# A two-layer mixture of experts on one Trainium2 core: two tiles of the first expert run from fixed rows, ahead of the last routing steps

## The chip, the core and the metric

One core of one Trainium2 chip. The metric is the device time of one execution in microseconds. Each core has TensorE (matrix products and turns, which are products with the identity), VectorE, ScalarE, GpSimd, SyncE and 16 DMA engines, which serve queues: q1 carries what SyncE issues, q10 what ScalarE issues, q0 what GpSimd issues.

## The reference

```
x   = attention(q, k pooled by 8, v pooled by 8)      # 2304 tokens of 512
lg  = x @ w_gate + log1p(exp(x @ w_noise)) * noise    # 8 experts
top = the two largest of each token, weights by softmax
for each expert e and each token that chose it:
    x2[token] += weight * (relu(x[token] @ w1[e]) @ w2[e])       # 512 -> 1024 -> 512
out = sum over 4 experts of p[e] * (relu(x2 @ w1b[e]) @ w2b[e])
```

## The kernel before

The work has three stages on one core, in one program per engine, tied together by semaphores.

**Stage A** goes over 18 tiles of 128 tokens. TensorE computes scores, turns, values and the gate's logits of a tile (`scores`, `e_turn`, `values`, `x_turn_a`, `logits`), VectorE the maxima, the normalisation (`post`) and, for a group of tiles, the choice of two experts (`select`) and the row of each token in its experts' lists (`places`, from the ranks that TensorE adds up in `ranks`). The groups are tiles 0-3, 4-7, 8-11, 12-14, 15-16 and 17 (`GROUPS`). A list of expert e lies in `x_sorted` in DRAM from row e * CAP + 128 on. GpSimd writes each token tile into it twice, by indirect DMAs (`scatter`, L500), one for each choice; tile t waits for `x_ps`, so that the transfers are spread. A ring of 10 tiles holds x (`x_sb`), with one semaphore per slot (`xs_out`).

When the last group is placed, TensorE adds up the counts (L835), and VectorE computes the first row (L1619-1627), the tile table (L1628-1652: which row each tile begins at), the classes and ranks by which 15 of 18 token tiles are sorted by their last expert (`SORTED`; L1655-1683, TensorE L839-841), the codes of the tiles (L1687-1702: expert, buffer, which pieces of weights to split), how many tiles the first block needs (`done_tiles`) and where each token's results lie in `y_sorted` (`y_places`, signal `posy_ok`).

**Stage B** goes over up to 43 row tiles of the lists (`TILES_B`; of these 40 are real with these inputs). Per tile: load 128 rows (ScalarE's queue, L1191 for tile 0, L1183 for others), turn (L859), split x into a high and a low part (ScalarE `x_hi` L1198, VectorE `x_lo` L1588), `up` (24 products in 3 passes, L878), relu (L1207), turn (L887), split h (`h_hi` L1216, `h_lo` L1708), `down` (24 products, L904), copy (L1719), store (L1223). `b_step(u)` on TensorE is: turn h of tile u, turn x of tile u+2, up of tile u+1, down of tile u. The weights come in four raw pieces of 1 MB per expert, through two buffers (`load_raw` on SyncE, L334, waits for `raw_used`), and are split into a high and a low part: for expert 0 ScalarE's `high_first` (L1147) and VectorE's `low_half` (L1581) do it during stage A, at the steps of `HIGH_AT` and `LOW_AT`; for the others GpSimd's `tile_b` (L638 and L641), piece r at the expert's tile r of the one before. GpSimd begins with this when `posy_ok` and all scatters are in, and after tile 0 it writes six token records in sorted order (`sort_records`, L615), after tile 3 nine more. The up of an expert's first tile waits for all four pieces.

In the gap the order of the programs is written out by hand. TensorE: ranks of the last groups, counts, `order_cols` products, `x_turn(0,0)`, `up(0,0)`, wait for the table, `x_turn(0,1)`, `b_step(0,0)`. VectorE: places, select, places, counts, table, `low_half(3, ...)`, `order`, `x_lo(0,0)`, codes, `x_lo(0,1)`, `done_tiles`, `y_places`, `b_step(0,0)`. SyncE: raw pieces 0 and 1, the probabilities, a fill of the lists' fronts from `w1` (L395), pieces 2 and 3, a fill of the tail of `y_sorted` by DRAM-to-DRAM copies (L401, 8 + 7 tiles of 256 KB), pieces of expert 1 and so on.

**Stage D** is the second layer in three blocks of 6 token tiles, with 7 products of halves in place of 8. The first block starts when 34 tiles (`DONE_TILES`) or fewer are stored; at the end each sorted token tile is written by GpSimd's indirect DMA (`store`, L621), the rest by SyncE's plain ones (L439).

```
            x_turn(0, 0)
            up(0, 0)
            pe.wait_ge(tab_ok, 1)
            x_turn(0, 1)
            for u in range(UNROLL_B):
                b_step(0, u)
```

Of the kernel before, what the change touches and what calls it, by code (L numbers as in the profile page):

```python
# [14 lines left out]
P = 128  # L15
# [22 lines left out]
TILES_B = 2 * N // P + EXPERTS - 1  # L38
# [4 lines left out]
SORTED = N // P - 3  # L43
# [39 lines left out]
def build(nc, q, k, v, w_gates, noise, w1, w2, probs, w1b, w2b, out):  # L83
# [5 lines left out]
    with ExitStack() as ctx:  # L89
# [49 lines left out]
        base8 = sb("list_base", [P, EXPERTS], F32, a_sc)  # L139
        noise_sb = sb("noise_sb", [P, NT, EXPERTS], F32, a_sc)  # L140
# [16 lines left out]
        t44 = sb("t44", [1, 18, TILES_B], F32, a_sc)  # L157
        t44i = sb("t44i", [1, 2, TILES_B], I32, a_sc)
        t448 = sb("t448", [1, 2, TILES_B, EXPERTS], F32, a_sc)
        q_sb = sb("qT", [P, 2, HEADS // 2, PAIR], F32, a_sc)  # L160
        kv = sb("kv_half", [P, 5, CHUNKS * POOL * HD // 2], F32, a_sc)
# [6 lines left out]
        nmax = sb("row_max", [P, 2, HEADS], F32, a_sc)  # L168
        ex = sb("exp_scores", [P, 2, HEADS * KEYS], F32, a_sc)
# [4 lines left out]
        aT = sb("x_sbT", [P, KD, P], F32, a_sc)  # L174
        a_sc.close()
# [68 lines left out]
        posy_ok, y_filled = S("y_positions_ready"), S("y_tail_filled")  # L244

# [29 lines left out]
        N_POOL_CONST = 15  # L275
# [44 lines left out]
        def _(sp):  # L320
# [69 lines left out]
            q_load(3)  # L390
            load_raw(0, 0, 0, None)
# [52 lines left out]
        def _(pool):  # L444
# [28 lines left out]
            pool.iota(jrow[:, :], pattern=[[1, TILES_B]], base=0, channel_multiplier=0,  # L473
                      allow_small_or_imprecise_dtypes=True).then_inc(c_pool, 1)
            pool.iota(jnext[:, :], pattern=[[1, TILES_B]], base=1, channel_multiplier=0,
                      allow_small_or_imprecise_dtypes=True).then_inc(c_pool, 1)
            pool.iota(jfirst[:, :], pattern=[[P, TILES_B]], base=0, channel_multiplier=0,
                      allow_small_or_imprecise_dtypes=True).then_inc(c_pool, 1)
            pool.memset(total_b[:, :, :], 0.0).then_inc(c_pool, 1)
            pool.iota(rec[:, :, REC - 1].bitcast(I32), pattern=[[P, NT]], base=0, channel_multiplier=1  # L480
# [12 lines left out]
            def scatter(g):  # L493
                pool.wait_ge(pos_ok, g + 1)
                first, end = GROUPS[g]
# [128 lines left out]
            def tile_b(g, u):  # L624
# [4 lines left out]
                for r in range(4):  # L629
                    with pool.If(code // (32 << r) % 2 > 0):  # L630
                        nslot = pool.snap((e + 1) % 2, min_val=0, max_val=1)
                        if not (isinstance(j, int) and j == 0):
                            pool.wait_ge(y_ps, first)
# [28 lines left out]
            with pool.Fori(1, SURE_GROUPS - 1) as g:  # L662
                for u in range(UNROLL_B):
                    tile_b(g, u)
# [19 lines left out]
            pool.wait_ge(y_ps, pool.value_load(tab2[0:1, 2:3], min_val=EXPERTS - 1, max_val=TILES_B - 1))  # L684
# [60 lines left out]
        def _(pe):  # L745
# [53 lines left out]
            def ranks(g):  # L799
# [3 lines left out]
                if g:  # L803
                    pe.wait_ge(pos_ok, g)
                dst = rank_cols[:, 0:EXPERTS * size]
                pe.matmul(dst, upper[:, :], mask_b[:, first:end, :], start=True, stop=False, skip_group_check=True)
                for j in range(1, size):
# [4 lines left out]
                          start=False, stop=True, skip_group_check=True).then_inc(rank_ps, 1)  # L812

# [15 lines left out]
            for g, (first, end) in enumerate(GROUPS[:-1]):  # L829
                if end + 3 >= NT + 2:  # L830
                    ranks(g)
# [1092 lines left out]
```

## Time and profile before

| | us |
|---|---|
| median of 3 runs | 1411.35 (1409.48 to 1411.98) |
| the profiled execution | 1418.43 |
| its span | 1416.7 |
| TensorE busy | 1348.5 (95%) |
| VectorE busy | 700.4 (49%) |
| GpSimd busy | 693.4 (49%) |
| ScalarE busy | 394.0 (28%) |

The profile follows one execution. The span is from its first to its last instruction; the execution's own time is 1.7 us more, and it lies 7.1 us over the median of the runs. "Granted clock" is TensorE's, as a share of 2.4 GHz: it is 1.0 or 0.5 at a time, and a stretch shows the mean. L is a line of the kernel, `<-` in brackets names who ended an idle time.

### The profile page before, as it was taken

To read this page: it belongs to the slowest core of one execution; us is meant where nothing else is said; L and a number is where in the kernel's file an instruction comes from. 1 tells how busy PE (TensorE), PEld (TensorE's weight loads), DVE (VectorE), ACT (ScalarE), POOL (GpSimd) and SP (SyncE) were. 2 spreads that over 40 slices of the span, in tenths; PEclk is the share of its full clock that TensorE was granted. 3 is DMA by queue.
4 is the path that set the end of the run, shared out by engine and by line. 5 is a ranking of instruction groups with operands and counts; after the bars stand their busy time and mean duration, and the time that the engine had idled before them with its cause. 6 is when DMAs were issued, how large, how long until landed. Compare 5 with 4: busy or idle time off the path is not lost.

```text
span 1416.7 us, 22026 instructions
## 1 busy us (share of the span) xinstructions
PE 1348.5 (95%) x6985; PEld 1186.7 (84%) x6986; DVE 700.4 (49%) x1292; ACT 394.0 (28%) x736; POOL 693.4 (49%) x464
## 2 busy tenths in 40 slices
PE   5992999999999999999999999999999999999997
PEld 4992788888888888878789889899899899989986
DVE  4786422222121222315876685855555655555564
ACT  2561212122212221413343443422222222222210
POOL 1244398274462928397877676442333222233202
PEclk9995999999999999999999999999999999999999
DMA  9948233252333426212323232210011000000002
GB/s 248 282 166 334 75 128 127 84 163 74 131 99 104 134 70 210 84 60 89 99 75 105 90 104 74 82 53 31 30 45 44 30 30 30 30 30 30 14 0 89
DMA packets 63604, 133.71 MB, mean 94 GB/s; under 512 B 5496, under 2 KB 23048, under 8 KB 63448
## 3 DMA queue, kind: packets, MB, share of 16 engines
q1 hardware_dynamic: 43320, 84.69, 18.5%
q0 software_dynamic: 8272, 26.49, 5.8%
q10 hardware_dynamic: 11952, 21.76, 4.7%
q8 instruction: 33, 0.54, 0.2%
q14 instruction: 27, 0.22, 0.1%
HBM read 108.22 MB, written 30.74 MB: 98 GB/s over the span
## 4 chain that ended last, share of the span: by engine, by line
PE 50%; DVE 2%; issue 1%; ACT 0%; DVEq 0%; ACTq 0%
PE banks L1025 26%; PE banks L998 23%; DVE hD L1809 1%; DVE acc L1852 0%; PE banks L984 0%; DVE block_sums L1826 0%; ACT hD L1337 0%; DVE acc L1855 0%; DVE block_sums L1832 0%; DVE x_ops L1805 0%; ACT acc L1227 0%; DVE block_sums L1823 0%; DVE x_sums L1786 0%; ACT unit_w L1359 0%; DVE block_sums L1820 0%
## 5 line engine op out<-in xcount | busy, mean ns | idle before, releaser
L1025 PE MATMUL banks<-unit_w,hD 128*128 128x512 f32 x1728 | 404.7, 391 | 3.2 <-DVE acc L1852 2.5
L1025 PEld LDWEIGHTS banks<-unit_w,hD 128*128 128x128 f32 x1728 | 322.2, 188 | 73.0 <-DVE acc L1852 7.1
L998 PE MATMUL banks<-x_ops,unit_w_hi 128*128 128x384 f32 x1344 | 342.3, 335 | 5.9 <-issue 2.6
L998 PEld LDWEIGHTS banks<-x_ops,unit_w_hi 128*128 128x128 f32 x1344 | 243.3, 188 | 11.5 <-issue 5.4
L1852 DVE SCALAR_TENSOR_TENSOR acc<-banks,sorted_record,acc 128x512 f32<-128x512 f32 x270 | 200.5, 748 | 104.4 <-PE banks L1025 101.5
L878 PE MATMUL banks<-expert_w,xT 128*128 (+1 forms) x960 | 230.7, 396 | 1.5 <-DVE xT L1588 1.5
L533 POOL TENSOR_TENSOR unit_w_lo<-raw_weights,unit_w_hi 128x512 fp32r<-128x512 f32 (+1 forms) x60 | 63.1, 1072 | 339.4 <-ACT unit_w_hi L1353 339.3
L904 PE MATMUL banks<-expert_w,hT 128*128 (+1 forms) x960 | 226.3, 392 | 2.7 <-issue 2.7
L998 PE MATMUL banks<-x_ops,unit_w_lo 128*128 128x384 f32 x672 | 225.1, 335 | 0.0
L904 PEld LDWEIGHTS banks<-expert_w,hT 128*128 128x128 f32 x960 | 181.2, 189 | 40.6 <-issue 3.0
L878 PEld LDWEIGHTS banks<-expert_w,xT 128*128 128x128 f32 x960 | 178.4, 189 | 38.5 <-issue 2.2
L1719 DVE COPY y_rows<-banks 128x512 f32<-128x512 f32 x40 | 27.7, 692 | 331.9 <-PE banks L904 331.9
L638 POOL TENSOR_TENSOR expert_w<-raw_weights,zeros 128x2048 f32 x28 | 100.8, 3600 | 168.6 <-PE banks L904 135.8
L641 POOL TENSOR_TENSOR expert_w<-raw_weights,expert_w 128x2048 f32 x28 | 128.8, 4602 | 5.2 <-POOL expert_w L638 5.2
L998 PEld LDWEIGHTS banks<-x_ops,unit_w_lo 128*128 128x128 f32 x672 | 126.1, 188 | 0.0
L1809 DVE SCALAR_TENSOR_TENSOR hD<-block_sums,hD 128x384 fp32r<-128x384 f32 x144 | 95.6, 692 | 28.6 <-ACT hD L1337 28.5
L1216 ACT CAST hT<-banks 128x512 fp32r<-128x512 f32 x80 | 43.0, 590 | 189.5 <-PE banks L887 189.5
L1207 ACT ACTIVATE h_rows<-banks 128x512 f32<-128x512 f32 x80 | 43.5, 595 | 180.4 <-PE banks L878 162.3
L537 POOL TENSOR_TENSOR unit_w<-raw_weights,unit_w 128x1024 fp32r<-128x1024 f32 x31 | 75.7, 2442 | 27.6 <-ACT unit_w L1359 27.6
L1335 ACT COPY block_sums<-banks 128x384 f32<-128x384 f32 x48 | 23.0, 480 | 205.1 <-PE banks L998 200.0
L1708 DVE TENSOR_TENSOR hT<-banks,hT 128x512 fp32r<-128x512 f32 x80 | 51.5, 686 | 49.1 <-ACT hT L1216 47.7
L533 POOL TENSOR_TENSOR unit_w_lo<-weight_sums,unit_w_hi 128x1024 fp32r<-128x1024 f32 x30 | 73.9, 2464 | 0.0
(232 smaller groups left out, 1278.0 us busy)
## 6 DMA issues: line engine op xcount, KB each, us to landing
raw_weights<-in_w SPq DMA_DIRECT2D x32, 1024.0 KB
raw_weights<-in_w1b SPq DMA_DIRECT2D x32, 512.0 KB
raw_weights<-in_w2b SPq DMA_DIRECT2D x32, 512.0 KB, 3.3
x_rows<-x_sorted ACTq DMA_DIRECT2D x43, 256.0 KB, 2.7
y_sorted<-y_rows ACTq DMA_DIRECT2D x40, 256.0 KB
qT<-in_q SPq DMA_DIRECT2D x3, 1152.0 KB, 23.0
kv_half<-in_k SPq DMA_DIRECT2D x5, 576.0 KB, 12.7
kv_half<-in_v SPq DMA_DIRECT2D x5, 576.0 KB, 12.3
```

Source lines behind the costliest of these rows:

```text
L533: ins = pool.tensor_tensor(lo, src, hi.bitcast(F32), ALU.subtract)
L537: pool.tensor_tensor(w2o[par][:, 1, :], raw[:, par, 1024:2048], w2o[par][:, 0, :].bitcast(F32), ALU.subtract).then_inc(w2_ok, 1)
L638: pool.tensor_tensor(hi, src, zeros[:, 0:1].to_broadcast([P, 2048]), ALU.add).then_inc(split_no, 1)
L641: pool.tensor_tensor(lo, src, hi.bitcast(F32), ALU.subtract).then_inc(raw_used[r % 2], 1)
L878: mm = pe.matmul(bank[n][:, :], xT[:, u % 2, st, c, :], wall[:, bass.ds(slot, 1), 0, mv, FF * c + 512 * n:FF * c + 512 * n + 512], start=( ...
L904: mm = pe.matmul(bank[5 + u % 2][:, :], hT[:, u % 2, st, c, :], wall[:, bass.ds(slot, 1), 1, mv, D * c:D * c + D], start=(t == 0), stop=(t ...
L998: mm = pe.matmul(dst[:, 0:HALF], (w1h, w1l)[st][par][:, b, c, :], x2o[blk][:, a, mv, c, :], start=(first and t == 0), stop=(t == 5), skip_ ...
L1025: mm = pe.matmul(bank[5 + t % 3][:, :], hD[:, buf, st, c, P * t:P * t + P], w2o[par][:, mv, D * c:D * c + D], start=(n == 0), stop=(n == 3 ...
L1207: r = act.activation(h_sb[:, 512 * n:512 * n + 512], bank[n][:, :], ACT.Relu)
L1708: d = dve.tensor_tensor(hT[:, u % 2, 1, 4 * n:4 * n + 4, :], bank[2 + n][:, :].rearrange("p (c r) -> p c r", c=4), hT[:, u % 2, 0, 4 * n:4 ...
L1809: dve.scalar_tensor_tensor(out=hD[:, buf, 1, m, at:at + HALF], in0=src, scalar=0.0, in1=hD[:, buf, 0, m, at:at + HALF].bitcast(F32), op0=A ...
L1852: dve.scalar_tensor_tensor(out=to, in0=bank[5 + t % 3][:, :], scalar=p, in1=to, op0=ALU.mult, op1=ALU.add).then_inc(acc_ok, 1)
```

## The change

Two tiles of expert 0 are taken from the front of its list at fixed rows (128 to 383) and computed with expert 0's weights while the last token tiles are still being routed; the tile table counts from the third tile on. The token tiles 0 to 11 (the first three groups) give these rows. If they have fewer than 256 tokens for expert 0, the rest of the 256 rows stays what a fill wrote (`early_filled`), and later tokens are placed behind (`late_base`, `early_count`). The loads of the two tiles are on SyncE's queue, behind the waits for the scatters of tiles 0 to 11 and ahead of expert 1's raw pieces. There are 45 row tiles in place of 43, 17 sorted token tiles in place of 15. `h_lo`, `y_copy`, `x_lo` of the early tiles stand among VectorE's table operations. Some buffers change places in memory.

```diff
+EARLY = 2
+EARLY_GROUPS = 3
-TILES_B = 2 * N // P + EXPERTS - 1
+TILES_B = 2 * N // P + EXPERTS - 1 + EARLY
-SORTED = N // P - 3
+SORTED = N // P - 1
-        HIGH_AT = {11: 0, 14: 1, 17: 2, 19: 3}
+        HIGH_AT = {11: 0, 14: 1, 17: 2}
 (SyncE)
             q_load(3)
+            sp.dma_start(x_sorted[P:P + EARLY_ROWS, :]..., w1[1]...[0:EARLY_ROWS, :]).then_inc(early_filled, 16)
             load_raw(0, 0, 0, None)
...
             load_raw(3, 0, 3, 1)
-            for i, (first, end) in enumerate(((DONE_TILES - 6, DONE_TILES + 2), (DONE_TILES + 2, TILES_B))):
+            for i, (first, end) in enumerate(((DONE_TILES - 6, DONE_TILES + 2), (DONE_TILES + 2, TILES_B - 1), (TILES_B - 1, TILES_B))):
                 sp.dma_start(y_sorted[first * P:end * P, :], w1[i]...).then_inc(y_filled, 16)
+            sp.wait_ge(sc_ps, NT)
+            for i in range(XS):
+                sp.wait_ge(xs_out[i], 32 * len(range(i, EARLY_TOKENS, XS)))
+            for j in range(EARLY):
+                sp.dma_start(xg[:, j, :], x_sorted[P + P * j:2 * P + P * j, :]).then_inc(xg_in[j], 16)
             with sp.Fori(1, EXPERTS) as e:
 (GpSimd)
                 pool.wait_ge(pos_ok, g + 1)
+                if g == 0:
+                    pool.wait_ge(early_filled, 16)
...
-            tile_b(0, 0)
-            pool.wait_ge(order_ok, 1)
-            pool.wait_ge(wts_ok, len(GROUPS))
-            pool.wait_ge(p_ok, 2)
-            sort_records(0, 6)
-            for u in range(1, UNROLL_B):
+            for u in range(EARLY, UNROLL_B):
                 tile_b(0, u)
-            sort_records(6, SORTED)
+            for g, (first, end) in enumerate(((0, 6), (6, 12), (12, SORTED))):
+                for u in range(UNROLL_B):
+                    tile_b(g + 1, u)
+                if g == 0:
+                    pool.wait_ge(order_ok, 1)
+                    pool.wait_ge(wts_ok, len(GROUPS))
+                    pool.wait_ge(p_ok, 2)
+                sort_records(first, end)
 (TensorE)
+                if s == EARLY_TOKENS + 4:
+                    early_count()
             x_turn(0, 0)
+            for g, (first, end) in enumerate(GROUPS[:-1]):
+                if end + 3 >= NT + 2:
+                    ranks(g)
             up(0, 0)
+            ranks(len(GROUPS) - 1)
+            x_turn(0, 1)
+            h_turn(0, 0)
+            count()
+            up(0, 1)
+            order()
+            down(0, 0)
+            h_turn(0, 1)
+            down(0, 1)
+            x_turn(0, EARLY)
             pe.wait_ge(tab_ok, 1)
-            x_turn(0, 1)
-            for u in range(UNROLL_B):
+            codes[EARLY] = load_code(pe, EARLY)
+            up(0, EARLY)
+            x_turn(0, EARLY + 1)
+            for u in range(EARLY, UNROLL_B):
                 b_step(0, u)
 (ScalarE)
             x_hi(0, 0)
+            high_first(3)
+            for g, (first, end) in enumerate(GROUPS):
+                if end + 3 >= NT + 2:
+                    second_exp(g)
+            relu(0, 0)
+            x_hi(0, 1)
+            h_hi(0, 0)
+            relu(0, 1)
+            h_hi(0, 1)
...
+            act.dma_start(xg[:, EARLY, :], x_sorted[bass.ds(row, P), :]).then_inc(xg_in[EARLY], 16)
             act.wait_ge(rows_ok, 1)
-            x_load(0, 1)
-            relu(0, 0)
-            x_load(0, 2)
-            x_hi(0, 1)
-            x_load(0, 3)
-            for u in range(UNROLL_B):
-                b_step(0, u, start=True)
+            x_load(0, EARLY + 1)
+            y_store(0, 0)
+            for u in range(EARLY):
+                x_load(1, u)
+            x_hi(0, EARLY)
+            x_hi(0, EARLY + 1)
+            relu(0, EARLY)
+            for u in range(EARLY, UNROLL_B):
+                b_step(0, u)
 (VectorE)
+            def late_base():
+                dve.wait_ge(early_ps, 1)
+                then(dve.tensor_tensor(bump8[:, 0, :], early8[:, :], count_cols, ALU.subtract))
+                then(dve.tensor_scalar(bump8[:, 0, :], bump8[:, 0, :], 0.0, None, ALU.max))
+                dve.tensor_tensor(base_late[:, :], base8[:, :], bump8[:, 0, :], ALU.add)
...
+                dve.sem_inc(early_ok, 1)
...
+                if s == EARLY_TOKENS + 5:
+                    late_base()
...
             for g in late:
                 places(g)
+            x_lo(0, 0)
             select(len(GROUPS) - 1)
+            low_half(3, 0)
             places(len(GROUPS) - 1)
+            x_lo(0, 1)
...
             dve.tensor_copy(first_row[:, :], front[0:1, 0:1]).then_inc(first_ok, 1)
+            low_half(3, 1)
+            h_lo(0, 0)
...
-            for half in range(2):
-                low_half(3, half)
...
             dve.tensor_copy(order_i[:, :], order_f).then_inc(order_ok, 1)
-            x_lo(0, 0)
+            h_lo(0, 1)
+            y_copy(0, 0)
...
-            x_lo(0, 1)
             done_tiles()
             y_places()
-            b_step(0, 0)
+            y_copy(0, 1)
+            x_lo(0, EARLY)
+            x_lo(0, EARLY + 1)
+            b_step(0, EARLY)
```

## Rows read from the trace of the kernel before

**Rows 1.** Busy time by stretch; columns PE, PEld, DVE, ACT, POOL, clock, DMA share, GB/s.
```profile
113.00:141.00 28.00, 3.63 (x30) 3.20 (x30) 17.75 (x73) 2.67 (x7) 11.90 (x12) 0.50 0.90 341
...
117.85:157.10 39.25, 13.90 (x71) 11.00 (x72) 21.29 (x95) 4.09 (x8) 8.09 (x9) 0.63 0.57 210
```

**Rows 2.** Timeline of TensorE; start, length, engine, line, count, idle before.
```profile
141.32 1.11 PE L859 MATMUL banks<-ident,x_rows 128*128 128x128 f32 x4 [10.14 <-DMA x_rows<-x_sorted]
...
155.18 5.74 PE L878 MATMUL banks<-expert_w,xT 128*128 x24
...
160.76 5.61 PE L904 MATMUL banks<-expert_w,hT 128*128 128x512 f32 x24
...
204.16 2.09 PE L878 MATMUL banks<-expert_w,xT 128*128 x8
```

**Rows 3.** Timeline of GpSimd, from the scatters to the fourth weight piece.
```profile
111.85 0.97 POOL L500 DMA_INDIRECT x_sorted<-x_sb,pos_int  x1 [0.30 <-issue]
...
127.40 0.97 POOL L500 DMA_INDIRECT x_sorted<-x_sb,pos_int  x1 [0.30 <-issue]
...
158.54 3.60 POOL L638 TENSOR_TENSOR expert_w<-raw_weights,zeros 128x2048 f32 x1 [30.17 <-issue]
...
194.15 3.60 POOL L638 TENSOR_TENSOR expert_w<-raw_weights,zeros 128x2048 f32 x1
197.94 4.61 POOL L641 TENSOR_TENSOR expert_w<-raw_weights,expert_w 128x2048 f32 x1 [0.19 <-POOL expert_w L638]
```

**Rows 4.** Timeline of VectorE: last selection, a low part of h, a copy.
```profile
117.89 0.18 DVE L1500 TENSOR_TENSOR noisy_logits<-noisy_logits,noise_sb 128x8 f32<-128x8 f32 x1
...
157.01 1.28 DVE L1708 TENSOR_TENSOR hT<-banks,hT 128x512 fp32r<-128x512 f32 x2
...
166.40 0.69 DVE L1719 COPY y_rows<-banks 128x512 f32<-128x512 f32 x1 [7.52 <-PE banks L904]
```

**Rows 5.** Waits of VectorE from 117.8 to 157.2; total, times, longest.
```profile
DVE xT L1588 <- ACT xT L1198: 10.7, 2, 5.8
DVE total_b L1519 <- DVE group_total L1516: 1.2, 1, 1.2
DVE cnt L1635 <- DVE cnt L1633: 1.0, 1, 1.0
```

**Rows 6.** Groups by line, 141 to 151.2 us: busy, mean ns, idle before.
```profile
L878 PE MATMUL banks<-expert_w,xT 128*128 128x512 f32 x24 | 7.3, 470 | 1.5 <-DVE xT L1588 1.5
```

**Rows 7.** Timeline of the DMA issues: y fill on SyncE, tile 0 on ScalarE.
```profile
106.25 1.73 SPq L401 DMA_DIRECT2D y_sorted<-in_w  x2
...
136.49 0.40 ACTq L1191 DMA_DIRECT2D x_rows<-x_sorted  x1
```

**Rows 8.** DMA queues, 100 to 106 us; packets, MB, share of 16 engines.
```profile
q0 software_dynamic: 240, 0.79, 34.5%
```

**Rows 9.** DMA queues, 110 to 122 us.
```profile
q1 hardware_dynamic: 263, 4.27, 94.7%
q0 software_dynamic: 121, 0.43, 9.3%
...
x_sorted<-x_sb,pos_int POOLq DMA_INDIRECT x9
```

**Rows 10.** DMA queues, 122 to 127 us, and time to landing.
```profile
q1 hardware_dynamic: 264, 1.00, 48.6%
q0 software_dynamic: 276, 0.91, 45.3%
...
x_sorted<-x_sb,pos_int POOLq DMA_INDIRECT x4, 9.0
```

**Rows 11.** Busy time by stretch around an early wait of TensorE, columns as in rows 1.
```profile
32.00:34.00 2.00, 0.49 (x4) 0.49 (x5) 0.10 (x1) 0.00 (x0) 0.00 (x0) 1.00 0.98 220
34.00:36.00 2.00, 2.00 (x13) 1.76 (x12) 1.23 (x2) 0.00 (x0) 0.00 (x0) 0.66 1.05 232
```

**Rows 12.** Timeline of the last stores.
```profile
1408.20 2.45 SPq L439 DMA_DIRECT2D out<-acc  x3
```

More of the change, by code:

```diff
@@ L631, in tile_b @@
                         nslot = pool.snap((e + 1) % 2, min_val=0, max_val=1)
-                        if not (isinstance(j, int) and j == 0):
-                            pool.wait_ge(y_ps, first)
+                        pool.wait_ge(y_ps, first)
                         src = raw[:, r % 2, :]
@@ L661, in _ @@
                            records[2 * BLOCK:SORTED * P, :].rearrange("(p t) r -> p (t r)", p=P)).then_inc(recs_in, 16)
-            with pool.Fori(1, SURE_GROUPS - 1) as g:
+            with pool.Fori(4, SURE_GROUPS - 1) as g:
                 for u in range(UNROLL_B):
@@ L812, in ranks, with early_count, count, order @@
                           start=False, stop=True, skip_group_check=True).then_inc(rank_ps, 1)
+            def early_count():
+                pe.wait_ge(tot_ok, EARLY_GROUPS)
+                pe.wait_ge(pos_ok, EARLY_GROUPS)
+                pe.matmul(count_cols, ones_b[:, :], total_b[:, EARLY_GROUPS % 2, :],
+                          start=True, stop=True).then_inc(early_ps, 1)
+            def count():
+                pe.wait_ge(tot_ok, len(GROUPS))
+                pe.wait_ge(pos_ok, len(GROUPS))
+                pe.matmul(count_cols, ones_b[:, :], total_b[:, len(GROUPS) % 2, :],
+                          start=True, stop=True).then_inc(cnt_ps, 1)
+            def order():
+                pe.wait_ge(class_ok, 1)
+                pe.matmul(order_cols, upper[:, :], class_b[:, :, :], start=True, stop=False, skip_group_check=True)
+                for j in range(1, SORTED + 1):
+                    mm = pe.matmul(order_cols[:, EXPERTS * j:], ones_b[:, :], class_b[:, 0:SORTED + 1 - j, :],
+                                   start=False, stop=j == SORTED, skip_group_check=True)
+                mm.then_inc(order_ps, 1)
             scores(0)
@@ L1169, in _ @@
                     high_first(HIGH_AT[s])
-            for g, (first, end) in enumerate(GROUPS[:-1]):
-                if end + 3 >= NT + 2:
-                    second_exp(g)
             softplus(len(GROUPS) - 1)
-            second_exp(len(GROUPS) - 1)
             codes = {}
@@ L1232, in first_copy, with b_step @@
                 act.copy(acc[1][:, n, :], first_bank(n)[:, :]).then_inc(x2T_ok, 1)
-            def b_step(g, u, start=False, rows=((), (), ())):
+            def b_step(g, u, rows=((), (), ())):
                 j = UNROLL_B * g + u
@@ L1239, in b_step @@
                 h_hi(g, u)
-                if not (start and u == 0):
-                    y_store(g if u else g - 1, (u - 1) % 4)
+                y_store(g if u else g - 1, (u - 1) % 4)
                 x_hi(g + (u + 2) // 4, (u + 2) % 4)
@@ L1589, in x_lo, with h_lo, y_copy @@
                                   xT[:, u % 2, 0, :, :].bitcast(F32), ALU.subtract).then_inc(bxT_lo, 1)
+            def h_lo(g, u):
+                j = UNROLL_B * g + u
+                dve.wait_ge(hT_hi, j + 1)
+                for n in range(2):
+                    d = dve.tensor_tensor(hT[:, u % 2, 1, 4 * n:4 * n + 4, :],
+                                          bank[2 + n][:, :].rearrange("p (c r) -> p c r", c=4),
+                                          hT[:, u % 2, 0, 4 * n:4 * n + 4, :].bitcast(F32), ALU.subtract)
+                d.then_inc(hT_lo, 1)
+            def y_copy(g, u):
+                j = UNROLL_B * g + u
+                dve.wait_ge(y_ps, j + 1)
+                if not (isinstance(g, int) and g == 0 and u < 2):
+                    dve.wait_ge(y_out[u % 2], 16 * (2 * g + u // 2))
+                dve.tensor_copy(y_sb[:, u % 2, :], bank[5 + u % 2][:, :]).then_inc(y_ok, 1)
             kv_pool(0, 0)
@@ L1696, in _ @@
             then(dve.tensor_copy(t44[:, 8, :], t44i[:, 1, :]))
+            then(dve.scalar_tensor_tensor(out=t44[:, 1, :], in0=behind[:, :, 0], scalar=float(EARLY), in1=t44[:, 1, :],
+                                          op0=ALU.mult, op1=ALU.add))
             then(dve.tensor_scalar(t44[:, 1, :], t44[:, 1, :], 1.0, None, ALU.max))
@@ L1757, in _ @@
             domain_weights()
-            for u in range(1, UNROLL_B):
+            for u in range(EARLY + 1, UNROLL_B):
                 b_step(0, u)
```

116 lines of the change are left out of this document (59 added, 57 removed).

## The prediction

> **What bounds the kernel now.** I read the windows of the start first: from 113 to 141 us TensorE works 3.63 us of 28 at a granted clock of 0.50, and from 141.3 on it multiplies with few breaks [rows 1, 2]. Whatever the change gives it must take from this gap, because the first expert network, once under way, runs at TensorE's pace: from the up of tile 1 (155.18, 5.74 us) to that of tile 5 (204.16) are four tiles, so 12.24 us each, of which up and down take 11.35 and turns the rest; two tiles are worth 24.5 us [rows 2]. Tile 5 is the first of expert 1; by its up both kernels have done the same products, and from there on they do the same, so **the start of up(5) is the mark by which I measure the change**.
>
> Three chains meet in the gap. VectorE goes from the last group's selection (117.89) to the y positions (done at 157.1) [rows 1, 4], but waited 10.7 us of these 39.2 for x, which TensorE turns and ScalarE casts [rows 5]. GpSimd issues scatters until 128.4, then waits for the y positions, and its four pieces of expert 1's weights begin at 158.54 and end at 202.55, 1.6 us before the mark [rows 3]. The queues are the third: the tile load is issued only at 136.49 though the last scatter was issued at 127.40, and TensorE can turn it at 141.3 [rows 2, 3, 7]. The DMA views say why. Up to 106 the scatter queue q0 had moved three scatters (0.79 MB of 0.26 each). The y fill is issued at 106.25; from 110 to 122 q1 moves 4.27 MB and q0 0.43 MB, though GpSimd had issued nine scatters in it; only from 122 on do they share (1.00 and 0.91 MB in 5 us) [rows 7 to 10]. Eight scatters, tiles 0 to 11's last, are 2.10 MB from 100 us on, and q0 reaches 0.79 + 0.43 + 0.91 = 2.13 MB at 127. So **tile 11's scatter, issued at 111.85, has landed only at about 127**.
>
> **The change, part by part.** The first two tiles are taken off the gap's end and put ahead of `ranks(4)` on TensorE, but they need rows that scatters of tiles 0 to 11 wrote.
>
> *When the early rows land (X).* SyncE waits for these scatters behind the y fill. The fill grows from 15 to 17 tiles, 3.75 to 4.25 MB; at q1's 4.27 MB in 12 us that is 1.4 us more, so it ends near 123.4. Against that, the raw load that shared with q0 from 122 is now issued behind the early loads. Alone, q0 gets about both shares, 1.91 MB in 5 us, so its missing 0.83 MB take 2.2 us: 125.6. From the queue's state to a load's issue and from there to TensorE's turn I take before's steps, about 1.0 and 4.8 us (136.49 to 141.32) [rows 2, 7]: X = 131.4, say **131**. Bounds: below, 112.8 + 4 + 2.8 = 119 or so if nothing starved; above, 134 if the three scatters of tile 12 on, already queued, take their full turn ahead.
>
> *From X to the y positions.* Relative to X: turn at half clock 1.1, `ranks(4)` and `places(4)` 1.4, and x's low half, so up(0,0) starts at 3.4 and takes before's 7.3 us for its 24 products, the first 3 us of them at the low clock [rows 6]: 10.7. `ranks(5)` stands behind it, so VectorE, which has finished the last selection and a weight half at 6.2, waits 4.9 us for it; `places(5)` and x's low half of tile 1 end at 13.1 and the counts come in. The steps that follow are small operations of 0.2 to 0.5 us, taken from before's timeline between the ends that the rows give, one by one, without its stalls. The first row 1.5, a weight half 1.2, h's low half of tile 0 1.3 [rows 4], the table's first part and the classes 4.1: 21.2. Meanwhile up(0,1) ended at 18.9 and TensorE stood for `order()`, which waits for the classes. `order()` 1.3 and down(0,0) 5.6 [rows 2] bring it to 28.3, turn and casts to 30.5. VectorE has the order at 26.4 and waits 4.1 us there for h of tile 1: its low half ends at 31.8, the copy of y (0.7) at 32.5 [rows 4], the tile table (4.4) at 37.0, done tiles and y places (1.6 + 2.0 and 0.7 for the added operations) at **X + 41.3**. The check from the other side: 39.2 - 10.7 us of waits = 28.5; VectorE's waits on itself while GpSimd issued scatters (1.2 and 1.0 are the longest [rows 5]) go, since its scatters lie elsewhere now, giving 26.3; added are two h halves 2.6, a copy 0.7, the small operations 1.1 and the two new waits 4.9 + 4.1: 39.7 from X + 2.5 on, 42.2, within 1 us of the other.
>
> *To the mark.* GpSimd starts 1.45 us after the positions (157.1 to 158.54) and splits four pieces at 8.37 us (194.15 to 202.55 holds one) without the six record scatters that lay between before: X + 41.3 + 1.45 + 33.5 = X + 76.3. TensorE's own way: up(0,2) waits for x's low half, which stands behind the y places and a copy in VectorE's order: X + 42.8, 5.74, the turn of x for tile 3, its cast, relu 2.3, then h's turn at 51.0, and from there two tiles and the turns, 25.7: X + 76.7. The two limits are level, so nothing is had by shortening one. The mark is at 131 + 76.7 = **207.7**, before 204.16: +3.5.
>
> *The clock.* TensorE now waits three times (2.3 us ahead of `order()`, 2.5 ahead of down(0,1), 4.6 ahead of up(0,2)). In the trace two microseconds with 0.49 busy (32 to 34) were followed by a granted clock of 0.66 [rows 11], while between the ups of tiles 0 and 1, which lie 4 us apart, nothing fell. Up(0,0) shows what low time costs: 7.3 us in place of 5.74 [rows 2, 6]. So 1.6 us a fall; I take one, +1.6. Bounds 0 and 4.8. [...]
>
> *The end.* 17 sorted tiles make tiles 3 and 4 of the last block go out by GpSimd's indirect store (about 1 us of issue, slower to land) in place of SyncE's plain ones, from 1408.20 on [rows 12]; the last tile stays plain. Bounds 0 and 1.5, I take 0.6. Two more empty tail steps on each engine, two more record scatters and `order()` products: the first 0.4 (0 to 1), the others lie under tiles with slack. The record scatters move between tiles 7 and 8, 11 and 12, 15 and 16; six are 7.6 us, four pieces 33.5, and five tiles last 61.2, so they fit. `late_base` (six operations, 1.2 us) comes before the last tile's x, and is hidden since X is later than all it delays. The early fill (0.5 MB at about 47 us) pushes weight loads that are needed at 80; free. Real tiles: 40 before; the inputs route 417 rows to expert 0 in its first 12 token tiles, over 256, so 40 again.
>
> Sum: +3.5 + 1.6 + 0.6 + 0.4 = **+6.1 us** on the profiled execution's 1418.4; on the median of the runs, 1411.35 (7 below it), that gives **1417.4**. This kernel's measurement can tell some 0.2%, 2.8 us, from no change.
>
> **The rivals.** (A) *The fill starves nobody when it counts, faster.* The place is SyncE's wait for tiles 0 to 11. The early rows then land at about 119, the chain of 76.7 ends at 195.7, and with a fall and the end the result is 8.5 less and 2.6 more, 5.9 less than 1411.35: 1405.5. The turning point is X = 125 (131 less 6.1). For it: q0 did move 0.43 MB during the fill and the three scatters before the fill were through by 106 [rows 8]. Against: every byte count above. The Trainium skill (DMA: Bandwidth & Descriptors, Anatomy of one DMA) gives a GpSimd-issued transfer 2.0 us and its bytes over 436 GB/s, an estimate of 2.6 us for 256 KB; with it the early rows would be in at 118 and the result near 1404. The trace's own landings of 9.0 us speak against it here [rows 10]. Chance 0.17.
> (B) *The chain is 4 to 5 us shorter than I add up, no change.* VectorE's waits on itself all go, no clock falls, X = 129: 1411 to 1414. Chance 0.20.
> (C) *More falls and a later X, slower still.* X at 134 puts the mark 6.5 later, three falls cost 4.8 and the end 1: 12.3 more than 1411.35, so 1423.7. Chance 0.15.
> (D) *The early tiles are padding or cost an extra tile*: expert 0 short of 256 rows, +12.2 us. Excluded by the 417 but for 0.01.
>
> **How the numbers follow.** The forecast as summed, 1414.2 to 1421, gets 0.47. Slower by over 0.2% is the forecast with (C) and (D), 0.63; same 0.20; faster 0.17. The range must take in part of (A) and most of (C): 1405 to 1423. The likeliest case's own range is 1414 to 1421.
>
> **What would show it.** The early x loads issued by SyncE at 125 to 128 and landing near 131, q0 nearly still until 123; y positions at 170 to 174; the first split piece right behind, four in a row; TensorE with 24 + 24 + 24 + 24 products between 134 and 169 and three waits; the mark near 208 to 210. The forecast is wrong if the first x turn comes before 125, or if up(5) does not stand at GpSimd's fourth piece or within 2 us of it.

## The result and the profile after

The changed kernel takes **1435.15 us** (median of 4 runs, 1430.53 to 1437.79) beside 1411.06 for the kernel before on the same chip: it is slower by 24.1 us. The ratio of the fast runs is 1.0151 (95% interval 1.0126 to 1.0176); the quotient of these two medians is 1.0171. The forecast was 1417.4: the sign came out, the size did not, and the time lies outside the range. The profile is of the fastest of the four runs (1430.53).

The page of the kernel after (its span, the busy tenths of TensorE in 40 slices, its clock):

```profile
span 1428.6 us, 22041 instructions
PE 1352.0 (95%) x6988; PEld 1188.3 (83%) x6989; DVE 711.2 (50%) x1302; ACT 393.6 (28%) x736; POOL 696.8 (49%) x470
...
PE   6995789999999999998999999999999999999997
```

In the stretch of [rows 1], busy time and clock are now these (columns as there):

```profile
113.00:141.00 28.00, 15.55 (x65) 12.44 (x66) 9.31 (x36) 5.22 (x9) 6.10 (x7) 0.67 0.55 213
```

TensorE works 15.55 of the 28 us in place of 3.63. Part of this is chance, since stage A ended some 7 us later in the first trace of before: in the repeated profiles below, the same stretch holds 13.47 in place of 6.10. The gap was filled as intended, and the time still went up. The timeline of TensorE tells where it went:

```profile
123.03 1.11 PE L897 MATMUL banks<-ident,x_rows 128*128 128x128 f32 x4 [14.93 <-DMA x_rows<-x_sorted]
...
125.80 8.39 PE L920 MATMUL banks<-expert_w,xT 128*128 128x512 f32 x24 [1.60 <-DVE xT L1675]
...
153.62 5.70 PE L948 MATMUL banks<-expert_w,hT 128*128 128x512 f32 x24 [2.58 <-DVE hT L1682]
...
164.23 8.00 PE L920 MATMUL banks<-expert_w,xT 128*128 x24 [4.47 <-DVE xT L1675]
...
200.19 7.16 PE L948 MATMUL banks<-expert_w,hT 128*128 x24 [6.48 <-issue]
207.19 1.04 PE L929 MATMUL banks<-ident,h_rows 128*128 128x128 f32 x8
208.42 5.74 PE L920 MATMUL banks<-expert_w,xT 128*128 x24
...
642.52 7.36 PE L948 MATMUL banks<-expert_w,hT 128*128 x24 [2.74 <-issue]
653.00 0.41 PE L1058 MATMUL banks<-x_ops,unit_w_hi 128*128 128x384 f32 x1 [3.12 <-issue]
654.52 0.48 PE L1058 MATMUL banks<-x_ops,unit_w_hi 128*128 128x384 f32 x1 [1.11 <-issue]
```

Three things answer to [rows 2]. The first x turn (X) is at 123.03. Up(5), the mark, is at 208.42, 85.4 us behind X and 4.3 us later than in the first trace of before. And stage D (L1058) does not start at the last down's end but 3.1 us behind it, with a second wait at once. The waits of 2.58 and 4.47 us and the two slow ups are near the forecast (2.5 and 4.6, and one fall of the clock); the 6.48 us ahead of down(3) are not.

The timeline of VectorE beside that wait, and then that of GpSimd:

```profile
186.97 0.69 DVE L1693 COPY y_rows<-banks 128x512 f32<-128x512 f32 x1 [8.51 <-PE banks L948]
187.57 1.80 DVE L1618 TENSOR_SCALAR top_sum<-top_diff_exp 128x2 f32<-128x2 f32 x1
189.40 0.17 DVE L1619 RECIPROCAL token_record<-top_sum 128x2 f32<-128x2 f32 x1
189.60 3.32 DVE L1620 TENSOR_TENSOR token_record<-top_diff_exp,token_record 128x2 f32<-128x2 f32 x1
...
193.22 4.39 DVE L1620 TENSOR_TENSOR token_record<-top_diff_exp,token_record 128x1 f32<-128x1 f32 x1
...
198.71 1.28 DVE L1682 TENSOR_TENSOR hT<-banks,hT 128x512 fp32r<-128x512 f32 x2
```

```profile
184.75 4.59 POOL L667 TENSOR_TENSOR expert_w<-raw_weights,expert_w 128x2048 f32 x1 [0.19 <-POOL expert_w L664]
189.30 3.60 POOL L664 TENSOR_TENSOR expert_w<-raw_weights,zeros 128x2048 f32 x1
193.09 4.50 POOL L667 TENSOR_TENSOR expert_w<-raw_weights,expert_w 128x2048 f32 x1 [0.19 <-POOL expert_w L664]
```

Three operations on one or two numbers per partition take 1.80, 3.32 and 4.39 us, and end at 189.37, 192.92 and 197.61, within 0.03 us of the ends of GpSimd's three splits (189.34, 192.90, 197.59). The low half of h, queued behind them, starts at 198.71, and down(3) needs it.

SyncE's issues in the gap (fill, then the early rows), and at the end the last accumulation and the last store:

```profile
98.19 2.76 SPq L418 DMA_DIRECT2D y_sorted<-in_w  x3
118.61 1.15 SPq L425 DMA_DIRECT2D x_rows<-x_sorted  x2
...
1418.49 0.75 DVE L1950 SCALAR_TENSOR_TENSOR acc<-banks,sorted_record,acc 128x512 f32<-128x512 f32 x1 [0.61 <-PE banks L1085]
1419.27 0.37 SPq L462 DMA_DIRECT2D out<-acc  x1
```

From the last accumulation's end (1419.24) to the span's end are 9.4 us; before it was 6.4.

### The profile page after: what moved, and what is told of

The parts are those of the page before. It is cut to its first block, busy times and chain, and to the rows that moved or that the text cites. A ratio compares the mean times of both kernels' runs of the same rounds, so it can differ in the third digit from the quotient of the medians.

```text
span 1428.6 us, 22041 instructions
## 1 busy us (share of the span) xinstructions
PE 1352.0 (95%) x6988; PEld 1188.3 (83%) x6989; DVE 711.2 (50%) x1302; ACT 393.6 (28%) x736; POOL 696.8 (49%) x470
## 4 chain that ended last, share of the span: by engine, by line
PE 50%; DVE 2%; issue 1%; ACT 0%; POOLq 0%; POOL 0%; DVEq 0%
PE banks L1085 26%; PE banks L1058 24%; DVE hD L1907 1%; DVE acc L1950 0%; PE banks L1044 0%; DVE block_sums L1924 0%; DVE acc L1953 0%; DVE block_sums L1930 0%; DVE x_ops L1903 0%; ACT acc L1275 0%; POOLq L95 0%; DVE x_sums L1884 0%; ACT hD L1402 0%; DVE x_sums L1886 0%; ACT hD L1406 0%
## 5 line engine op out<-in xcount | busy, mean ns | idle before, releaser
L1058 PE MATMUL banks<-x_ops,unit_w_hi 128*128 128x384 f32 x1344 | 343.5, 336 | 9.9 <-issue 6.8
L1058 PEld LDWEIGHTS banks<-x_ops,unit_w_hi 128*128 128x128 f32 x1344 | 244.1, 188 | 14.3 <-issue 9.0
L920 PE MATMUL banks<-expert_w,xT 128*128 (+1 forms) x960 | 234.4, 401 | 6.3 <-DVE xT L1675 6.3
L948 PE MATMUL banks<-expert_w,hT 128*128 (+1 forms) x960 | 228.2, 394 | 11.8 <-issue 9.2
L1058 PE MATMUL banks<-x_ops,unit_w_lo 128*128 128x384 f32 x672 | 225.8, 336 | 0.0
L1058 PEld LDWEIGHTS banks<-x_ops,unit_w_lo 128*128 128x128 f32 x672 | 126.5, 188 | 1.3 <-issue 1.3
```

The lines of the kernel that those rows point to most:

```text
L920: mm = pe.matmul(bank[n][:, :], xT[:, u % 2, st, c, :], wall[:, bass.ds(slot, 1), 0, mv, FF * c + 512 * n:FF * c + 512 * n + 512], start=( ...
L948: mm = pe.matmul(bank[5 + u % 2][:, :], hT[:, u % 2, st, c, :], wall[:, bass.ds(slot, 1), 1, mv, D * c:D * c + D], start=(t == 0), stop=(t ...
L1058: mm = pe.matmul(dst[:, 0:HALF], (w1h, w1l)[st][par][:, b, c, :], x2o[blk][:, a, mv, c, :], start=(first and t == 0), stop=(t == 5), skip_ ...
```

## The experiments

Times are medians; the kernel before had 1411.6, 1412.8 and 1412.1 us in the three sets of runs (e1 to e4; e5, e7, e8, e10; e11 to e14). "From X to the mark", "last down to last accumulation" and "end" are read from each run's timeline as above.

### The two kernels again

No edit. The kernel before, profiled once more:

> The kernel before, profiled a second time, to see how far its first profiled execution (1418.43 us against a median of 1411.4) speaks for it. Theory A (the first profile had a stage A that was some 7 us too long by chance: last logits at 115.06 against 108.13 in the profile of the changed kernel, whose stage A is the same up to there): the last logits now end near 108, the product of tile 5 that was at 204.16 starts near 197, and the time is near 1411. Theory B (the change itself shortens stage A by some 7 us, through the moved fill or the moved scatters): the last logits end near 115 and the product of tile 5 starts near 204 again.

```profile
134.68 1.11 PE L859 MATMUL banks<-ident,x_rows 128*128 128x128 f32 x4 [15.43 <-DMA x_rows<-x_sorted]
...
199.94 5.73 PE L878 MATMUL banks<-expert_w,xT 128*128 x24
...
633.73 7.35 PE L904 MATMUL banks<-expert_w,hT 128*128 x24 [2.74 <-issue]
640.92 0.51 PE L998 MATMUL banks<-x_ops,unit_w_hi 128*128 128x384 f32 x2
```

1413.94 us, a single run, span 1412.2; the last logits' products end at 107.0, the mark is at 199.9 and not at 197, since this time X lies 65.3 us ahead of it in place of 62.8. Theory A holds: the trace that the prediction used had a stage A that was longer by chance.

> The changed kernel again, for a second profile and for its spread on the chip of these runs. Theory A (the first profile, 1430.5 us, was its fastest run; the others lie 3 to 7 us above it because the gap at the start of stage D and the TensorE clock there vary with the fetches of code): the median is 1434 to 1436 and the gap from the last down's end to the steady products of stage D is 5 us or more, against 4.7 in the first profile. Theory B (they vary through stage A and the first x turn, 123.0 to 126.1 so far): the first x turn is at 125 or later and the transition is as it was.

1434.59 us, span 1432.4, with X at 125.09 and the mark at 211.27 (X + 86.2). Both theories hold in part: from the last down to the last accumulation it takes 778.5 us in place of 776.7, and X and the mark are later by 2 to 3 us. Between these two repeated profiles the spans differ by 20.2 us: 11.3 up to the mark, -0.6 from there to the last down, 6.4 from there to the last accumulation (778.5 against 772.1), 3.0 at the end (9.4 against 6.4). These are the parts to explain.

### The weights' operations ahead of the splits

```diff
@@ VectorE, after order_ok
+            for g in late + [len(GROUPS) - 1]:
+                pair_weights(g)
+            domain_weights()
             h_lo(0, 1)
...
             y_places()
+            rest_rows()
...
             b_step(0, EARLY)
-            for g in late + [len(GROUPS) - 1]:
-                pair_weights(g)
-            domain_weights()
```

`rest_rows` is the last part of `domain_weights`, the copies that need the y positions.

> The changed kernel with VectorE's small operations on the weights of the late tokens moved ahead, to where GpSimd has no split running; nothing is left out. Theory 1 (each of these operations of 0.16 us is held until the instruction that runs on GpSimd ends, 8 us in all, and so the cast h_lo of the first tile of list 3 comes late and TensorE waits 6.5 us before down(3)): that wait goes, the product of tile 5 starts about 8 us earlier relative to the first x turn (now 85.4 after it, then some 77), and the time falls by 6 to 9 us, to 1427 to 1429. Theory 2 (rival: what sets the start of down(3) is TensorE's own slow clock and GpSimd's splits of x, and VectorE's lateness is cover): 83 to 86 us after the first x turn, the time within 2 us of 1435. The small operations themselves should take 0.16 to 0.3 us each by theory 1.

```profile
151.64 0.16 DVE L1621 TENSOR_SCALAR top_sum<-top_diff_exp 128x2 f32<-128x2 f32 x1
...
152.04 0.16 DVE L1623 TENSOR_TENSOR token_record<-top_diff_exp,token_record 128x2 f32<-128x2 f32 x1
...
152.50 0.16 DVE L1623 TENSOR_TENSOR token_record<-top_diff_exp,token_record 128x1 f32<-128x1 f32 x1
```

1426.05 us (ratio to before 1.0101, interval 1.0086 to 1.0117), 8.5 less than the changed kernel in its second set. The same operations take 0.16 us, down(3) follows its h turn without a wait, and the mark is at 203.14, 77.2 behind X (125.90). Theory 1 holds: it had some 77 from X to the mark; the time lies 1 us below its 1427 to 1429.

### Which operations are held

Made in the kernel of the section above:

```diff
             b_step(0, EARLY)
+            for n in range(6):
+                dve.reciprocal(psum_p[:, 2 * n:2 * n + 2, :], pinv[:, 2 * n:2 * n + 2, :])
```

> The kernel with the weights' operations moved ahead (e2_weights_early), and at their old place, beside GpSimd's splits, six reciprocals of 128x2 f32 from SBUF to SBUF whose result nobody reads. Theory P (what is held beside a running split is a VectorE operation that wants the port pair that it shares with GpSimd: one with two inputs in SBUF, or TENSOR_SCALAR and copies of f32 in their fast mode; RECIPROCAL, of which two in the changed kernel took 0.17 us beside a running split, is not): each takes 0.14 to 0.2 us and the time is that of e2_weights_early, 1424 to 1428. Theory S (rival: any operation of VectorE on SBUF alone is held until GpSimd's instruction ends, and the two reciprocals slipped in between two splits): the first is held for some 2 us and another for 3.5 to 4.5 us, and the time rises by 3 to 8 us over e2_weights_early.

```profile
188.51 0.46 DVE L1861 RECIPROCAL prob_sum<-prob_inv 128x2 f32<-128x2 f32 x6
```

GpSimd's split ran from 186.04 to 190.65, so all six stood beside it; together they took 0.46 us, and the time is 1424.07. Theory P holds for what was tried: it is not every operation on SBUF that waits. The Trainium skill (SBUF — State Buffer, SBUF: two separate sides) holds that VectorE and GpSimd share a port pair, which an operation of VectorE in a two-port mode, or with two inputs in SBUF against a GpSimd operation that reads SBUF, and one of GpSimd take for a whole instruction, the loser blocked. The traces agree: the two TENSOR_TENSOR and the f32 TENSOR_SCALAR were held for 3.2, 4.2 and 1.6 us; RECIPROCAL with its one input was not, nor in this run, beside splits, the copy (0.69 us at 187.91) and the two low halves of h (1.29 us at 189.89), which read PSUM. That the TENSOR_SCALAR ran in a two-port mode no run shows.

### The fill behind the early rows

```diff
-            for i, (first, end) in enumerate(((DONE_TILES - 6, ...
-                sp.dma_start(y_sorted[first * P:end * P, :], ...).then_inc(y_filled, 16)
             sp.wait_ge(sc_ps, NT)
...
                 sp.dma_start(xg[:, j, :], ...).then_inc(xg_in[j], 16)
+            for i, (first, end) in enumerate(((DONE_TILES - 6, ...
+                sp.dma_start(y_sorted[first * P:end * P, :], ...).then_inc(y_filled, 16)
```

> The changed kernel with SyncE's fill of the end of y_sorted put behind its two loads of the early rows; nothing is left out. Theory 1 (the fill's large packets, issued at 98.2, share the DMA engines with the scatters of x and the copy of raw weights, so that the scattered rows land late and the first x turn comes 24.8 us after the fill is issued): without it in front the first x turn comes 6 to 12 us earlier than now, at 111 to 119 in place of 123 to 126, the product of tile 5 follows with 80 to 86 us after it, and the time falls by 5 to 11 us, to 1424 to 1430. Theory 2 (rival: the landings are late through the raw weights of SyncE and the indirect scatters themselves, the fill is a small part): the first x turn stays within 3 us of 124 and the time within 3 us of 1435.

```profile
109.60 0.85 SPq L422 DMA_DIRECT2D x_rows<-x_sorted  x2
110.50 1.83 SPq L424 DMA_DIRECT2D y_sorted<-in_w  x3
```

1422.80 us (ratio 1.0066, interval 1.0053 to 1.0079), 11.8 less than the changed kernel. The early rows' loads are issued at 109.60 in place of 120.76, X is at 112.62 in place of 125.09. The lines of the DMA view from 98 to 124 us say why (number of scatters issued, and median us to landing), first of the changed kernel in its first profile, then of this one:

```profile
x_sorted<-x_sb,pos_int POOLq DMA_INDIRECT x11, 13.4
```

```profile
x_sorted<-x_sb,pos_int POOLq DMA_INDIRECT x15, 7.6
```

Theory 1 holds, the gain of X a little over its bound. From X to the mark it still takes 86.5.

The same edit in the kernel before (the fill behind three of expert 1's raw pieces):

> The kernel before with the same fill put behind three quarters of the raw weights of expert 1; nothing is left out. It is the control of the run above: if the fill delays the scatters, the kernel before pays for it as well. Theory 1: its first x turn (134.7 in the second profile, 14 us behind its last scatter) comes 3 to 8 us earlier and the time falls by 3 to 8 us, to 1403 to 1408. Theory 2 (its first tile waits for the order of the scatters and for VectorE's positions, and the fill's packets are over by then): the time stays within 1.5 us of 1411.5.

1407.40 us (ratio 0.9963, interval 0.9949 to 0.9976): X moves from 134.68 to 130.69, the median by 5.4. The profiled run, 1411.09, was one of the slower of the ten. Theory 1 holds. So the delay by the fill is no fault of the change; but the change moved a wait for the scatters to where the fill costs 12 us instead of 4 to 5.4.

### Tile steps: 43, 41, and GpSimd's alone

```diff
-TILES_B = 2 * N // P + EXPERTS - 1 + EARLY
+TILES_B = 2 * N // P + EXPERTS - 1
-DONE_TILES = TILES_B - (SORTED - 6)
+DONE_TILES = 34
```

> The changed kernel with 43 tile steps as before instead of 45 (three empty steps in place of five for this input; for other inputs it would lack room for two tiles). Theory 1 (each two further empty steps keep TensorE's instruction stream busy for a fetch of code more, and the first product of stage D starts 3 us behind the last down, at a slower clock): the gap between the last down and the first product of stage D goes from 3.1 us to below 0.5 us and the time falls by 4 to 5.5 us, to 1430 to 1431. Theory 2 (rival: what stage D waits for at its start is the last tile's store or the weights of stage D, and the empty steps lie under it): the gap stays near 3 us and the time stays within 1.5 us of 1435.

```profile
642.85 7.36 PE L948 MATMUL banks<-expert_w,hT 128*128 x24 [2.74 <-issue]
650.05 0.51 PE L1058 MATMUL banks<-x_ops,unit_w_hi 128*128 128x384 f32 x2
```

1425.50 us (ratio 1.0100, interval 1.0085 to 1.0116), 9.1 less than the changed kernel, so more than theory 1 had. The gap is gone; from the last down to the last accumulation it takes 772.0 us. The profiles with five empty steps have 776.4 to 781.4 there, so the pair costs 4.4 to 9.4, 6.4 in the two repeated profiles. The rest lies ahead of the last down: the mark is at 209.05 in place of 211.27, X at 123.97 in place of 125.09, and the fill is two tiles shorter.

> The kernel before with 41 tile steps instead of 43 (one empty step in place of three for this input; for other inputs it would lack room for two tiles). The three sizes 41, 43 and 45 then stand side by side. Theory 1 (TensorE's sequencer runs through the empty steps while the last down's products run, and only what is longer than that shows; with three it is just hidden): no gain, the time within 1 us of 1411.5, and no gap ahead of stage D either way. Theory 2 (each pair of empty steps costs its 4.7 us wherever it stands): the time falls by 4 to 5 us, to 1407. The wait of 2.74 us ahead of the last down stands in both; if the empty steps caused it too, it shrinks here.

 (the kernel before with `EXPERTS - 3`)

1411.43 us beside 1412.82 (interval 0.9982 to 1.0001; one of the eleven runs took 1530.45), 771.3 us from the last down. Theory 1: with three empty steps the tail is already covered.

By then the traces offered another cause. GpSimd goes through the tail steps too, and its operands for stage D are ready only about when stage D starts. Its first sum, in the timelines of the kernel before with 41 steps, of that with 43, and of the changed kernel:

```profile
582.43 0.74 POOL L553 TENSOR_TENSOR unit_sums<-raw_weights 128x256 f32<-128x256 f32 x1 [7.38 <-issue]
```

```profile
589.50 0.73 POOL L553 TENSOR_TENSOR unit_sums<-raw_weights 128x256 f32<-128x256 f32 x1 [11.01 <-issue]
```

```profile
604.05 0.73 POOL L580 TENSOR_TENSOR unit_sums<-raw_weights 128x256 f32<-128x256 f32 x1 [14.76 <-PE banks L948]
```

That is 1.8 to 1.9 us for each empty step. So GpSimd alone was given 43:

```diff
-            for j in range(SURE_TILES, TILES_B):
+            for j in range(SURE_TILES, TILES_B - 2):
                 tile_b(*divmod(j, UNROLL_B))
```

> The changed kernel with 45 tile steps on every engine but GpSimd, which goes through 43 (the last two are empty for this input). Theory G (GpSimd is the one that the two further empty steps hold: from its last fetch to the first sum for stage D it takes 7.4, 11.0 and 14.7 us with one, three and five empty steps, and its 51.5 us of operands for stage D end 3.6 us behind the last down in place of level with it): the idle time ahead of that first sum is 11.0 us again, stage D starts within 0.5 us of the last down's end at full clock, and from the last down's start to the last accumulation it takes 772 us as with 43 steps, against 776.4 to 781.4 with five. The time falls by 5 to 9 us, to 1426 to 1430. Theory T (rival, the one first held: TensorE's own fetches and tests in its tail steps hold the first product): TensorE still has its five, so the gap stays at 3 us or more and the time within 1.5 us of 1434.6.

```profile
601.21 0.73 POOL L580 TENSOR_TENSOR unit_sums<-raw_weights 128x256 f32<-128x256 f32 x1 [11.01 <-issue]
...
650.37 2.36 POOL L590 TENSOR_TENSOR unit_w_lo<-unit_sums,unit_w_hi 128x1024 fp32r<-128x1024 f32 x1
```

```profile
645.39 5.73 PE L948 MATMUL banks<-expert_w,hT 128*128 x24 [2.74 <-issue]
655.34 0.66 PE L1058 MATMUL banks<-x_ops,unit_w_hi 128*128 128x384 f32 x1 [4.21 <-issue]
658.23 0.48 PE L1058 MATMUL banks<-x_ops,unit_w_hi 128*128 128x384 f32 x1 [2.23 <-issue]
```

1434.44 us: nothing gained, and **theory G falls**. GpSimd was through at 652.7, and TensorE still began stage D at 655.34, 4.2 us behind the last down. What is left are the empty steps of the other engines, TensorE's own most likely: the profile shows nothing that it waited for, and from the last down's start to stage D's first product it takes 9.95 us here, 6.4 in the run with 43 steps whose down was as short (below), 1.8 us a step again. No run gave 43 steps to TensorE alone, so ScalarE's and VectorE's are not excluded. The rest of the cost comes behind the first product: from it to the last accumulation this run takes 768.1 us, the second profile of before 764.9. A second wait takes 2.23 us of it, and then the products run at a granted clock of 0.55 for 3.1 us, where before had 1.0.

### 15 sorted row tiles

```diff
-SORTED = N // P - 1
-DONE_TILES = TILES_B - (SORTED - 6)
+SORTED = N // P - 3
+DONE_TILES = 34
```

> The changed kernel with 15 of the 18 row tiles sorted, as before, instead of 17; the tiles and the early work stay. Theory 1 (the end of the changed kernel is 2.9 us longer from the last accumulation to the last byte because GpSimd's last indirect stores of sorted rows end it where SyncE's three plain stores ended it before): the last accumulation to the end of the span takes 6.4 to 7 us in place of 9.4 and the time falls by 2 to 3 us, less what the sooner start of the combine was worth. Theory 2 (rival: 17 sorted tiles let the combine begin with ready rows and win time in stage D, which the end only gives back in part): the time rises by 1 to 4 us. Stage D from its first product to the last accumulation tells how much: now 1419.2 less 653.0, that is 766.2 us.

```profile
1419.17 3.05 SPq L462 DMA_DIRECT2D out<-acc  x3
...
1421.11 0.75 DVE L1950 SCALAR_TENSOR_TENSOR acc<-banks,sorted_record,acc 128x512 f32<-128x512 f32 x1 [0.61 <-PE banks L1085]
```

1432.07 us (interval of the ratio 1.0131 to 1.0159), 2.5 less; three plain stores are back, and from the last accumulation's end (1421.86) to the span's end are 6.4 us. Theory 1 holds, and stage D itself is no longer (765.7 us from its first product against 766.2): the two more sorted tiles brought nothing there.

### All together

> Every mend together: the changed kernel with the fill behind the early rows' loads, the weights' operations ahead, 43 tile steps and 15 sorted row tiles (for other inputs two tiles short of room). What is left of the change is the early work alone. Theory (the four costs add up, each as it was measured alone): first x turn at 112.6, the product of tile 5 starts 77.2 us later at 190, the last down 434 us after that, the last accumulation 772 us after its start, the end 6.4 us and 1.8 us later: 1404, less 1 to 4 us by the medians of the runs, so 1400 to 1404, below the kernel before with its fill moved (1407.4). Rival (the mends overlap, since after one is made another wait decides at the same place, such as the raw weights of the next expert or GpSimd's splits): 1407 to 1415.

```profile
110.64 1.12 PE L897 MATMUL banks<-ident,x_rows 128*128 128x128 f32 x4 [3.79 <-DMA x_rows<-x_sorted]
...
186.32 5.72 PE L920 MATMUL banks<-expert_w,xT 128*128 x24
...
620.10 5.71 PE L948 MATMUL banks<-expert_w,hT 128*128 x24 [2.74 <-issue]
626.53 0.58 PE L1058 MATMUL banks<-x_ops,unit_w_hi 128*128 128x384 f32 x2 [0.73 <-issue]
```

**1399.25 us** (ratio 0.9924, interval 0.9905 to 0.9943), by the medians 12.8 us below the kernel before and 8 below that with its fill moved; by the ratios, since two of the six runs took 1404.2 and 1406.6, it is 11 and 5 to 6. The mends add up. The two early tiles are worth the smaller of these once their surroundings fit, since moving the fill helps the kernel before too; but with 43 steps and this bound the kernel would lack room for some other inputs.

> The mends that hold for every input: 45 tile steps and 17 sorted row tiles as in the changed kernel, the fill and the weights' operations moved, and on GpSimd the last four tile steps under one test of whether the first of them is real. Theory G (empty steps cost through GpSimd alone): the same as the run before but for the end, which is 2.9 us longer, so 1403 to 1407. Theory T (TensorE's empty steps cost too): 4 to 8 us more, 1408 to 1414.

```diff
-            for j in range(SURE_TILES, TILES_B):
+            for j in range(SURE_TILES, TILES_B - 4):
                 tile_b(*divmod(j, UNROLL_B))
+            with real(pool, load_code(pool, TILES_B - 4)):
+                for j in range(TILES_B - 4, TILES_B):
+                    tile_b(*divmod(j, UNROLL_B))
```

The moved fill and weights' operations are as above.

1413.43 us (interval 0.9994 to 1.0014): level with before. Theory T fits once more, with the same engines left open: with 45 steps on TensorE stage D starts 11.4 us behind the last down's start, 4.2 us of it a wait, and the stretch to the last accumulation is 778.8. Even GpSimd's saving was small: passing over four steps in one jump left 10.7 us ahead of its first sum. Of the kernels that hold for every input, the kernel before with its fill moved is the fastest, 1407.4.

## Why the prediction was wrong

**When the early rows land: right.** X was put 24.8 us behind the issue of the fill (131 less 106.25); it was 24.8 and 26.0 (123.03 less 98.19, 125.09 less 99.12). The mechanism, that the fill starves the scatters, is shown by moving it. Rival (A) had no part in the kernel as it was.

**From X to the y positions: right.** They ended at X + 39.7 (forecast 41.3), GpSimd's fourth piece at X + 74.6 (76.3), and without the held operations the mark stood at X + 77.2 (76.7).

**From X to the mark: the step that failed.** "Splits four pieces ... without the six record scatters that lay between before" was taken as a gain for GpSimd and no loss to anyone. Before, GpSimd stood idle while VectorE computed the weights of the records, because it waited for them. With the scatters moved back, it splits during these operations and holds them until each split ends. X + 76.7 became X + 85.1 to 86.5 in the traces with these operations at their place. The only thing I had asked of VectorE's operations was their length in the trace of before, measured beside an idle GpSimd. That stood in the trace of before:

```profile
167.01 0.16 DVE L1540 TENSOR_SCALAR top_sum<-top_diff_exp 128x2 f32<-128x2 f32 x1
...
167.41 0.17 DVE L1542 TENSOR_TENSOR token_record<-top_diff_exp,token_record 128x2 f32<-128x2 f32 x1
...
170.05 0.98 POOL L615 DMA_INDIRECT token_records<-token_record,token_order  x1 [3.12 <-DVE sorted_record L1436]
```

**The mark itself: luck.** It was put at 207.7 and stood at 208.42 in the first profile, because two differences cancelled: stage A ran shorter than in the trace of before, so the fill was issued 8.1 us sooner (98.19 against 106.25), and X to the mark took 8.7 us longer. Both signs of being wrong that the prediction named came up all the same. Up(5) stood 10.8 us behind GpSimd's fourth piece, where 2 us were allowed. X came at 123.03, before 125, though by the shorter stage A and not by rival (A)'s mechanism.

**The clock.** One fall was taken, 1.6 us. In the first profile the product behind the wait of 2.58 us ran at full speed (5.70), those behind 4.47 and 6.48 us slowly (8.00 and 7.16), so 2.3 and 1.6 us: two falls, 3.9 us, and the second belongs to the wait that was not foreseen. In the second profile all three were slow, 7.32, 7.34 and 8.46 us behind waits of 2.58, 2.85 and 7.19, which is 6.2 us over their full-speed lengths, more than the 4.8 of rival (C)'s three falls. X to the mark was still the same within 1 us, since a slow down(1) shortened the wait behind it. So one fall was too few, and the count varies from run to run. Rivals (B) and (C) had the wrong mechanism: neither a shorter chain nor a later X, but a wait of its own.

**Two more empty tail steps: taken at 0.4, bounded at 1; they cost 6.4.** They were priced as if the last down covered any number. It covers three, and where it ran at full speed even these left 0.73 us; five it does not cover. The bound from above needed the row that was there, GpSimd's 11 us of idle time with three empty steps, and the question of what covers it, though the run above shows that it is not GpSimd's own time that sets the start.

**The end: taken at 0.6, bounded at 1.5; it cost 3.0** between the profiles and 2.5 between the medians.

**The profiled execution.** The sum was made in a trace whose stage A ran some 7 to 8 us long, and whose X lay 2.4 us closer to the mark than in the repeat. Put against the repeated profile of before, the same steps give a mark of 99.12 + 24.8 + 76.7 = 200.6, 0.7 later and not 3.5, hence 3.3 us in all. Measured were 20.2. The difference of 16.9 is X 1.2 later, 9.5 from X to the mark, 6.0 for the tail, 2.4 for the end, less the 1.6 of the clock counted apart and 0.6 between the mark and the last down.

## What to carry over

A move that fills one engine's idle time may take away the cover under which another engine's short operations ran: look at what stood beside them, above all at VectorE operations with two inputs in SBUF beside long GpSimd ones. A wait that is moved forward must be looked at with the large transfers issued ahead of it; here the order of two DMA issues on SyncE was worth 12 us. Padding this loop with empty steps cost nothing only as long as the last product covered them; the size of that cover is read from the trace before steps are added.

## What had not been expected of the hardware

An operation of 0.16 us on VectorE took up to 4.39 us beside a GpSimd split, and six reciprocals beside such a split took 0.46 us in all. An empty tail step cost 1.8 to 1.9 us on GpSimd and, from the start of the last down to stage D's first product, 1.8 us on TensorE's side. Jumping over four such steps at once saved GpSimd little: 10.7 us, where one empty step had 7.4. This jump was not looked into further.
